# Attention and two feed-forward layers on one core: first block with its own weight places, later stores, two X buffers, split token loads

## The reference

```python
q_s = exp(q - max(q, -1)); q_s /= sum(q_s, -1) + 1e-9       # over the 64 of head_dim
k_s = exp(k - max(k, 2));  k_s /= sum(k_s, 2) + 1e-9        # over the 576 of seq
attn = q_s @ (k_s^T @ v)                                   # 8 batches, 8 heads, 576 x 64
x = attn as 4608 tokens x 512
x = (silu(x @ w_gate) * (x @ w_val)) @ w_out               # 512 -> 1536 -> 512
out = max(x @ w1, x @ w2, x @ w3) @ w_out2                 # 512 -> 768 -> 512
```

## Time and profile before

| what | us |
|---|---|
| median of 3 runs | 1587.88 (1584.59 to 1588.61) |
| profiled execution, its own time | 1585.31 |
| its span | 1583.5 |
| TensorE busy | 1502.0 (95%) |
| VectorE, ScalarE, POOL busy | 812.2, 544.7, 653.9 |

### The profile page before, as it was taken

How to read it: one execution, slowest core, us unless ns; L and a number is a source line. 1 busy time by engine, 2 the same in 40 slices (tenths; PEclk the granted TensorE clock), 3 DMA queues, 4 the chain that set the end, 5 groups by cost and what they waited for, 6 DMA issues and landing times.

```text
span 1583.5 us, 20727 instructions
## 1 busy us (share of the span) xinstructions
PE 1502.0 (95%) x7002; PEld 1242.5 (78%) x7002; DVE 812.2 (51%) x1344; ACT 544.7 (34%) x996; POOL 653.9 (41%) x523
## 2 busy tenths in 40 slices
PE   8677879999999999999999999979999999999999
PEld 7566657787787888888888888868888888888898
DVE  6444335676575654755446454633453443443444
ACT  4334234353443432433233222523422322322322
POOL 5344367655643333433143231687751251241121
PEclk9888999999999999999999999989999999999999
DMA  8767567686776667565565655286685575575585
GB/s 231 257 187 245 185 212 249 205 285 216 250 242 196 212 190 250 183 201 161 182 215 186 215 166 153 74 317 213 253 289 176 168 262 175 168 236 174 168 304 200
DMA packets 180903, 334.56 MB, mean 211 GB/s; under 512 B 13376, under 2 KB 68672, under 8 KB 173120
## 3 DMA queue, kind: packets, MB, share of 16 engines
q1 hardware_dynamic: 175616, 323.80, 62.5%
q10 hardware_dynamic: 5184, 9.44, 1.9%
HBM read 256.90 MB, written 76.28 MB: 210 GB/s over the span
## 4 chain that ended last, share of the span: by engine, by line
PE 81%; POOL 6%; DVE 4%; issue 3%; ACT 2%; DMA 2%; SPq 1%; ACTq 0%; DVEq 0%; POOLq 0%
PE round L1560 12%; PE round L1563 12%; PE round L1562 12%; PE y_bank L1588 8%; PE y_bank L1590 8%; PE y_bank L1589 8%; PE third_bank L1560 5%; PE third_bank L1563 5%; PE third_bank L1562 5%; PE att_bank L1493 2%; DMA kt_sb<-k_t 1%; PE round L1453 1%; PE att_bank L1498 1%; PE round L1454 1%; PE round L1455 1%
## 5 line engine op out<-in xcount | busy, mean ns | idle before, releaser
L598 POOL TENSOR_TENSOR h<-hid,h 128x512 fp32r<-128x512 f32 (+1 forms) x156 | 201.7, 1294 | 461.3 <-ACT h L1081 460.8
L1560 PE MATMUL round<-xops,wring 128*128 128x512 f32 (+1 forms) x930 | 358.6, 386 | 19.4 <-POOL wring L582 9.7
L1563 PE MATMUL round<-xops,wring 128*128 128x512 f32 (+1 forms) x930 | 354.3, 381 | 0.0
L1562 PE MATMUL round<-xops,wring 128*128 128x512 f32 (+1 forms) x930 | 354.0, 381 | 0.0
L1363 DVE TENSOR_TENSOR y_sb<-y_sb,y_bank 128x512 f32<-128x512 f32 x232 | 158.3, 684 | 234.1 <-PE y_bank L1590 233.8
L1560 PEld LDWEIGHTS round<-xops,wring 128*128 128x128 f32 x930 | 175.7, 189 | 55.7 <-issue 15.0
L1563 PEld LDWEIGHTS round<-xops,wring 128*128 128x128 f32 x930 | 175.7, 189 | 33.6
L1562 PEld LDWEIGHTS round<-xops,wring 128*128 128x128 f32 x930 | 175.9, 189 | 31.7
L1081 ACT ACTIVATE h<-hid 128x512 fp32r<-128x512 f32 (+1 forms) x156 | 95.4, 612 | 191.2 <-DVE hid L1324 118.8
L1588 PE MATMUL y_bank<-h,wout 128*128 128x512 f32 x384 | 151.8, 395 | 0.0
L1590 PE MATMUL y_bank<-h,wout 128*128 128x512 f32 x384 | 149.8, 390 | 0.0
(11 more groups left out here) (153 smaller groups left out, 2634.9 us busy)
## 6 DMA issues: line engine op xcount, KB each, us to landing
wring<-kept SPq DMA_DIRECT2D x216, 512.0 KB, 4.0
wout<-kept_o SPq DMA_DIRECT2D x36, 1024.0 KB, 6.2
wring<-kept SPq DMA_DIRECT2D x108, 256.0 KB, 3.4
stage<-x_dram SPq DMA_DIRECT2D x32, 512.0 KB, 6.3
kept<-wring SPq DMA_DIRECT2D x9, 1792.0 KB, 9.5
kept<-wring SPq DMA_DIRECT2D x12, 1024.0 KB, 6.1
raw<-w_g SPq DMA_DIRECT2D x21, 512.0 KB, 4.7
x_dram<-stage SPq DMA_DIRECT2D x16, 576.0 KB, 3.6
```

Of the source, the lines that this page charges most:

```text
L598: pool.tensor_tensor(h[:, t, 1, 0:cols], hid[:, t, 0:cols], h[:, t, 0, 0:cols].bitcast(F32), ALU.subtract).then_inc(h_lo_ready, 1)
L1560: pe.matmul(dst[:, 0:g.cols], hi, x1, start=(i in (1, 5) and c == 0), stop=False, skip_group_check=True)
L1562: pe.matmul(dst[:, 0:g.cols], hi, x2, start=False, stop=False, skip_group_check=True)
L1563: mm = pe.matmul(dst[:, 0:g.cols], lo, x1, start=False, stop=(c == 1), skip_group_check=True)
```

## The change

Seven parts. (1) The 24 gate and val units get places in xops (operands 2 to 4, unit_tiles) instead of wring, and unit_stage moves from raw to hid, c22 and p5; raw and wring are thereby free from the start, so load_raw and load_weights of groups 0 and 1 go at gates 2 and 3, load_raw(2) at gate 7, and first_weights (combinations and splits of groups 0 and 1, combination of group 2) at gates 5 to 7. (2) keep_unit stands one step of j later. (3) x_out has two buffers, one for each half, each with a semaphore. (4) load_x is split into two halves of two transfers; the first half of pair 0 goes at gate 6, the second behind val 10; each later first half goes one group or more ahead of the second. split_x 0 goes at gate 7, split_x 2 at gate 10; a split now waits for its own half. (5) Batches 1 and 2 are spread over 31 slots instead of 26. (6) Group 0 runs its products in the order 1, 2, 5, 6, 3, 7, 4, with second 10 behind product 1 and second 11 behind product 2; h has four places in the first block. (7) sum_x(5) and load_x(5) of pair 4 move: sum_x(5) behind product 1 of group 55, the halves of load_x(5) behind product 1 of group 53 and product 6 of group 54.

```diff
+FIRST_SEVEN = (1, 2, 5, 6, 3, 7, 4)
-X_SOURCE = (0, 1, 2, 3, None, 4, 5)
+X_SOURCE = (0, 2, 1, 3, None, 4, 5)
...
-    timed += [(3 * 9 + 1.7, ("load_x", 0)), (3 * 10 - 0.4, ("sum_x", 0))]
-    timed += [(3 * 10 + 0.6 + k, ("split_x", 0, k)) for k in range(5)]
-    timed += [(3 * 9 + 1.8, ("first_weights", 0)), (3 * 10 + 0.7, ("first_weights", 1)),
-              (3 * 11 - 0.3, ("first_weights", 2))]
-    timed = spread(timed, (1, 2), 26)
+    timed += [(3 * 6 + 0.2, ("load_x", 0, 0)), (3 * 7 + 0.2, ("split_x", 0, 0)), (3 * 10 + 0.2, ("split_x", 0, 2)),
+              (3 * 10 + 1.2, ("load_x", 0, 1)), (3 * 11 - 0.2, ("sum_x", 0))]
+    timed += [(3 * 11 + 0.2 + k, ("split_x", 0, o)) for k, o in enumerate((1, 3))]
+    timed += [(3 * (5 + k) + 0.1, ("first_weights", k)) for k in range(3)]
+    timed = spread(timed, (1, 2), 31)
+    timed.remove((3 * (F1 - 1) + 1.5, ("second", F1 - 2)))
...
+                if n == 0 and i in (1, 2):
+                    units.append(("second", F1 - 3 + i))
...
-            timed += [(1.5, ("split_x", 0, 5)), (2.5, ("split_x", 0, 6))]
+            timed += [(1.5 + k, ("split_x", 0, o)) for k, o in enumerate((4, 5, 6))]
...
-            if pair < 3:
-                timed.append((where["product", final - 2, 6] + 0.3, ("load_x", pair + 1)))
-                timed.append((where["product", final - 1, 1] + 0.3, ("sum_x", pair + 1)))
-            else:
-                timed.append((where["product", final - 7, 1] + 0.3, ("load_x", pair + 1)))
-                timed.append((where["product", final - 6, 1] + 0.3, ("sum_x", pair + 1)))
+            early = 0 if pair < 3 or pair == PAIRS1 else 5
+            timed.append((where["product", final - 3 - early, 1] + 0.3, ("load_x", pair + 1, 0)))
+            timed.append((where["product", final - 2 - early, 6] + 0.3, ("load_x", pair + 1, 1)))
+            timed.append((where["product", final - 1 - early, 1] + 0.3, ("sum_x", pair + 1)))
...
-        unit_stage = raw[:, :, :, :].rearrange("p a (u b) e -> p (a u) (b e)", b=2)
+        unit_stage = [hid[:, 2, :], hid[:, 3, :], c22[:, :], p5[:, :]]
+        unit_tiles = [xops[:, 2 + place // 2, place % 2, :, :] for place in range(6)]
-        x_out = spare[:, 0:PAIRS * HALF].rearrange("p (n t) -> p n t", t=HALF)
+        x_out = [spare[:, first:first + PAIRS * HALF].rearrange("p (n t) -> p n t", t=HALF)
+                 for first in (4 * BLOCK, 8 * BLOCK)]
...
-                    if e[1] == 0:
-                        combine_weights(0)
-                    elif e[1] == 1:
-                        split_weights(0, 1)
-                    else:
-                        split_weights(0, 2)
-                        combine_weights(1)
+                    if e[1]:
+                        split_weights(e[1] - 1, 1)
+                        split_weights(e[1] - 1, 2)
+                    combine_weights(e[1])
...
-                    sp.wait_ge(x_stored, 32 * min(3 + 2 * pair, BATCH))
+                    last = (first + cols - 1) // HALF
+                    for n in (last - 1, last):
+                        sp.wait_ge(x_stored[n % 2], 16 * (n // 2 + 1))
...
-                elif e[0] == "gate" and e[1] == 10:
-                    load_raw(0)
-                    load_raw(1)
+                elif e[0] == "gate" and e[1] in (2, 3):
+                    load_raw(e[1] - 2)
+                    for piece in range(3):
+                        load_weights(e[1] - 2, piece)
+                elif e[0] == "gate" and e[1] == 7:
+                    load_raw(2)
...
-                    if e[1] + 2 < F1:
-                        keep_unit(3 * (e[1] + 2))
+                    if e[1] + 1 < F1:
+                        keep_unit(3 * (e[1] + 1))
...
-            for n in range(6):
+            for n in range(3):
                 keep_unit(n)
...
-                    if p == 0 and not (b == 0 and half == 0):
-                        dve.wait_ge(x_stored, 32 * b + 16 * half)
-                    if b == 0 and half == 1:
-                        dve.wait_ge(x_lo_first, p + 1)
+                    if p == 0 and b:
+                        dve.wait_ge(x_stored[half], 16 * b)
...
-                if j >= 2:
-                    act.wait_ge(first_h_used, j - 1)
-                act.activation(h[:, j % 2, 0, :], hid[:, j % 2, :], ACT.Copy).then_inc(first_h_hi, 1)
+                if j >= 4:
+                    act.wait_ge(first_h_used, j - 3)
+                act.activation(h[:, j % 4, 0, :], hid[:, j % 2, :], ACT.Copy).then_inc(first_h_hi, 1)
...
-                elif o >= 5:
-                    act.wait_ge(val_done, F1)
-                act.wait_ge(x_in, 64 * (pair + 1))
+                elif o >= 2:
+                    act.wait_ge(val_done, min(F1 - 4 + o, F1))
+                    if o < 5:
+                        for place in (2 * o - 4, 2 * o - 3):
+                            act.wait_ge(unit_kept[place], 32 * 4)
+                act.wait_ge(x_in[0 if o in (0, 2) else 1], 32 * (pair + 1))
```

More of the change, by code:

```diff
@@ L236, in whole_order @@
             n = group_of(s, kind)
-            for i in SEVEN:
+            for i in SEVEN if n else FIRST_SEVEN:
                 if i == 4:
@@ L400, in unit_weights @@
                 return wout[:, j % 4, :, :]
-            half, place = divmod(unit_place(n), 3)
-            flat = wring[:, half, :, :, :].rearrange("p s a e -> p (s a e)")
-            return flat[:, place * 1024:(place + 1) * 1024].rearrange("p (a e) -> p a e", a=2)
+            return unit_tiles[unit_place(n)]
         rounds = [bank(f"round{n}") for n in range(3)]
@@ L465, in program @@
         item_out_act, item_out_dve = sem("item_out_act"), sem("item_out_dve")
-        x_stored = sem("x_stored")
+        x_stored = [sem(f"x_stored{n}") for n in range(2)]
         block = ctx.enter_context(nc.Block())
@@ L507, in transfers, with hi_count @@
                        if not made(m) or (GROUPS[m].layer == 1 and piece < 3))
+        def hi_count(pair, o):
+            return op_hi[o % 2], (4 - o % 2) * pair + o // 2 + 1
         def wout_made(s):
@@ L702, in store_x @@
                 first = (2 * b + half) * HALF
-                sp.dma_start(x_dram[:, :, first:first + HALF], x_out[:, :, :]).then_inc(x_stored, 16)
+                sp.dma_start(x_dram[:, :, first:first + HALF], x_out[half][:, :, :]).then_inc(x_stored[half], 16)
             def after_item(b, n):
@@ L766, in load_weights @@
                     sp.wait_ge(done[PIECES[piece][0 if made(n) else -1]], n - 1)
-                else:
-                    sp.wait_ge(val_done, F1 - 1 + n)
-                    for place in range(3):
-                        sp.wait_ge(unit_kept[3 * n + place], 32 * 4)
                 if made(n):
@@ L817, in keep_wout, with load_x @@
                 sp.dma_start(kept_o2[STEPS[s].number], wout[:, first:first + 2, :, :].bitcast(F32)).then_inc(wout_kept, 16)
-            def load_x(pair):
-                cols, first = COLS[pair], FIRST_TOKEN[pair]
+            def load_x(pair, half):
+                cols = COLS[pair]
+                first = FIRST_TOKEN[pair] + half * cols
                 if pair:
@@ L829, in load_x @@
                 src = x_dram if pair < PAIRS1 else x2_dram
-                for n, place in enumerate((0, 2, 4, 5)):
-                    t, c = divmod(n, 2)
-                    at = first + t * cols
-                    sp.dma_start(stage[:, place, :, 0:cols], src[:, 2 * c:2 * c + 2, at:at + cols])\
-                      .then_inc(x_in, 16)
+                for c, place in enumerate((0, 1) if half == 0 else (4, 5)):
+                    sp.dma_start(stage[:, place, :, 0:cols], src[:, 2 * c:2 * c + 2, first:first + cols])\
+                      .then_inc(x_in[half], 16)
             def store_first(m):
@@ L1092, in split_weights @@
                             act.wait_ge(w_kept[n % 2], 16 * made_before(n, n % 2))
-                    else:
-                        act.wait_ge(val_done, F1 - 1 + n)
-                        for place in range(3):
-                            act.wait_ge(unit_kept[3 * n + place], 32 * 4)
                 if piece == 0:
@@ L1168, in next_after @@
                         split_h(n, TILE[i])
-                    if i in (5, 2, 6) and n + 1 < NGROUPS and made(n + 1):
+                    if i in (5, 2, 6) and 0 < n < NGROUPS - 1 and made(n + 1):
                         split_weights(n + 1, (5, 2, 6).index(i))
```

71 lines of the change are left out of this document (34 added, 37 removed).

## The result

| | median, us | range | profiled execution: its time, its span |
|---|---|---|---|
| before (5 runs beside it) | 1586.88 | 1582.02 to 1588.61 | 1585.31, 1583.5 |
| after (5 runs) | 1573.29 | 1571.76 to 1575.45 | 1575.45, 1573.7 |

A forecast was written before the change was run, and what follows sets the result against it. TensorE, 95% busy, was bound by idle stretches and lower clock. Span 1583.5 - 23.6 (up to product 7 of group 0) - 8.6 (layer 2) = 1551.3; with overhead and adjustment to the median, 1556 us, range 1546 to 1565.

The forecast's parts named there:

- Other pairs: 0: Token loads and sums of pairs 1 to 3 and 6 to 8: no TensorE wait, so 0 us change.
- Step (3): Batches 1 and 2 over 31 slots: 10.9 us of products added, filling idle time by 5.5 us (bounds 0 and 10.9).
- Step (2): Later stores beside batches 1 and 2: shorter k_max waits, -8.3 us of idle time (bounds -3 and -12.3).
- Step (4): Weights of groups 0 to 2 beside batch 2: 13.6 us more on POOL, +4.5 us showing (bounds 0 and 13.6).
- Step (5): Lower clock beside batches 1 and 2: less of it as idle time falls, -5 us (bounds 0 and -13).
- (1): Two X buffers: copy of X 4 no longer waits for a store, -1.3 us; the stretch starts at 40.5.
- rival (a): Batches bound by vector chains and POOL, not order: batch 2 ends at 206, time 1575 us; chance 0.18.
- The hand-over: End of batch 2 to product 7 of group 0: 34.4 us (23.1 to 40), product 7 23.6 us earlier.
- The other chain starts at the same place: copy 0.45: Hand-over chain of copy, store and token loads, starting where batch 2's last item ends: 12.0 us until x lands.
- The 3.5 us added for lower clock: Hand-over: waits at products 2 and 5 bring the clock down, adding 3.5 us up to product 7.
- Layer 2: Group 51 wait goes, -11.1 us; group 56 loses 2.5: together -8.6 us (bounds -4.3 and -11.1).

The follow-up runs named there:

- the other execution with this order: The new kernel with both token-load halves of pairs 6 to 8 put back where they were before; 1565.98 us, ratio 0.9873.

## Why the prediction was wrong in size

The direction and the places were right, the size was not: 13.6 of 31.9 us.

**"Other pairs: 0" failed, and is the largest part: 8.3 us behind group 56, and the 6.1 us at the end of this section.** It was argued from POOL's being free ahead of the sums, and left out two things: that the second half of the loads of pairs 6 to 8 moves three products later in SP's queue, and that h splits are queued behind the sums on POOL. Putting those loads back gives 7.3 us (8.3 in the profiles, from product 1 of group 56 to the end). The prediction's own words were "the second later than all four now"; the product behind which it stands was never set against the time at which the sums start.

**Step (3), "part of the 30.0 us of idle time is filled", failed.** It took -5.5 on its own. Three slots more on the kernel before lengthen the stretch by 9.8 us and fill nothing. Within the range given (0 to -10.9) the end "none of it" was right for that kernel.

**Step (2), the stores, was mis-sized:** -8.3 of idle time forecast; the lengths with and without differ by 4.1 and 6.2 us, the medians by 5.0 and 6.5, and the waits for k_max by only 1.7 in each pair. The 5.6 us wait for k_max went in the new kernel, and SP no longer stands for units; but waits of up to 3 us for k_max stayed and SP stands for X copies. With late stores alone that wait is still 4.6 us.

**Step (4), the weights on POOL, was wrong as a constant.** Forecast +4.5; 0.7 to 3.4 at 31 slots, 12.4 to 14.5 at 26. Steps (3) and (4) are not two terms that can be added. The wide spread is worth 8.4 us (6.8 by the ratios) when the weights are beside the batch; with none of them there, three slots more gave nothing, and two more cost 9.7.

**Step (5) and the sum.** (1) held: the copy of X 4 no longer waits for a store, and the stretch starts at 40.0 (forecast 40.5). Together (1) to (5) should have brought the last X item 4.7 us earlier; it came 3.2 later. The stretch ends at 194.0 instead of 186.4: 4.3 us are idle time (33.3 against 29.0) and 3.8 are (5), busy time at the lower clock that did not go (9.7 more against 5.9), less 0.5 at the start. Of these two (5) is partly luck: in the other execution with this order, with a clock of 0.92, the busy time is 116.7, which is the 116.9 that the forecast makes (111.0 + 5.9), and the last X item comes at 191.0. The idle time is 34.6 there, so it is the sure part. That is rival (a) in part, chains and not order bound the batches: it forecast 206, the forecast 186.4, the runs 191 to 194.

**The hand-over was right in its sum, 34.4 against 34.0 from the start of val 10, by luck: two errors cancelled.** "The other chain starts at the same place: copy 0.45" overlooked VectorE's queue: the copy ran 5.5 us behind its matmul. (The kernel before had it too, 4.6 us: 190.72 to 195.35.) Putting it first gave 4.8 us of the hand-over, and of the median. It did not show in the sum: x was 3.5 us later than forecast, product 2 lost 6.78 us instead of 3.3, and with that product 5 came at 222.9, when its split was about done, so that its 3.5 us fell away; product 6 then waited 1.03. The 3.5 us added for lower clock are about right: 26.39 us of busy time for 23 us of work.

**Layer 2** held: 10.6 at group 51 (forecast 11.1), 2.3 lost at group 56 (forecast 2.5).

**The 6.1 us between product 7 and batch 5 stay open.** They fall under the same "Other pairs: 0". They are systematic: against the kernel before, the new one and the nine made from it lose 5.8 to 9.1 us there, the three made from the kernel before -0.2 to 2.2. TensorE is idle for 10.8 us between the landmarks instead of 8.1, nearly all for links of batches 3 to 5, and busy for 263.9 instead of 260.5, at a mean clock of 0.99 instead of 1.00. The later stores, the 31 slots, the place of the first weights and the loads of pairs 6 to 8 are not the cause: the kernels that take these back one at a time still lose 5.8 us or more. Left are, above all, the two X buffers, the split loads of pairs 1 to 3, the order of group 0 and the four places of h; none of these was tried alone.

## What to carry to other kernels

An in-order queue sets a result's time by what stands ahead of it, also when its input is long there: for each step on the path of a hand-over, read the event behind which its engine issues it. Here one copy brought ahead of one multiplication gave 4 to 5 us of the median, and half a token load three products later cost 7.3. A load that is split is two moves, each with its own due time. And work put beside a chain of small steps has no fixed price: some 13 us of POOL cost 3 us or less in a spread order and 12 to 14 in a dense one, so such terms are to be tested in pairs. Last, look at the granted clock before a landmark is put down to an edit: two executions with the same order were 3 us apart by it.

## What the runs showed of the hardware

The subtraction of combine_weights that took 2.13 us at the hand-over the earlier trace rows takes 1.26 to 1.31 us in all three places beside batch 2, as here on POOL of the new kernel, and 2.16 in one place of the kernel that puts it back at the hand-over (1.29 in another). So moving it made it no dearer in itself, though VectorE is busy for 71 of 154 us there; the rest of step (4) must lie in the queue, which was not tested apart.

```profile
114.87 1.29 POOL L571 TENSOR_TENSOR combos<-raw 128x512 f32<-128x512 f32 x1
...
130.61 1.26 POOL L571 TENSOR_TENSOR combos<-raw 128x512 f32<-128x512 f32 x1
...
147.27 1.31 POOL L571 TENSOR_TENSOR combos<-raw 128x512 f32<-128x512 f32 x1
```

What VectorE does at that moment tells the two apart. At both slow places (212.38 in the kernel before, 222.84 with the late weights) it is in the middle of a split of x, whose two inputs, stage and xops, are both in SBUF. It ends at 213.37 and 223.89, 1.0 us behind the start of POOL's instruction, and POOL's ends 1.1 us behind that:

```profile
212.14 1.23 DVE L1368 TENSOR_TENSOR xops<-stage,xops 128x1024 fp32r<-128x1024 f32 x1 [5.06 <-ACT xops L1124]
```

```profile
222.68 1.21 DVE L1370 TENSOR_TENSOR xops<-stage,xops 128x1024 fp32r<-128x1024 f32 x1
```

At the three fast ones VectorE runs no such instruction while POOL's does its work: there are multiplications that take one input from the matmul's result (115.57, 147.03), a reduction with one input (131.68), and a split of h that begins at 148.42, 0.16 us before the third ends. The Trainium skill, SBUF — State Buffer, section "SBUF: two separate sides", says that a VectorE instruction with two SBUF inputs and a POOL instruction that reads SBUF take one port pair by turns, each to its end. The two slow places agree with it, and the three beside the batch do not test it.

The wait of 5.48 us in pair 6 was followed by the lower clock: six y matmuls take 0.63 to 0.76 us instead of 0.39, and the 5.5 us cost 7.3. Behind the wait of 2.09 us (group 56) the matmuls stay at 0.39. The length of the wait does not decide it. One wait for wring, at the same product in both kernels, was followed by full clock in the kernel before (2.27 us) and by matmuls of 0.63 us in the new one (2.25 us; granted clock 0.51 from 412.3 to 415.8):

```profile
423.63 0.47 PE L1560 MATMUL third_bank<-xops,wring 128*128 128x512 f32 x1 [2.27 <-POOL wring L578]
423.93 0.40 PE L1562 MATMUL third_bank<-xops,wring 128*128 128x512 f32 x1
```

```profile
412.32 0.73 PE L1561 MATMUL third_bank<-xops,wring 128*128 128x512 f32 x1 [2.25 <-POOL wring L586]
412.86 0.63 PE L1563 MATMUL third_bank<-xops,wring 128*128 128x512 f32 x1
```

Nor does the first matmul behind a wait tell it: the y product of the kernel with its sums behind product 7 took 0.47 us behind its wait of 2.24, and those from 0.65 us later on took 0.63. And a wait of 2.19 us, 6.6 us behind one of 1.54 (kernel with the copy first), was followed by 0.79.
